# Attention softmax: exponential and row sums in one ScalarE instruction from PSUM, earlier q and k loads, fewer idle products

## What is computed

```python
scores = scale * np.matmul(q, k.transpose(0, 1, 3, 2))
mask_local = (rel >= 0) & (rel < 32)
mask_strided = (rel >= 0) & (pos[None, :] % 32 == pos[:, None] % 32)
# heads 0 to 3 local, 4 to 7 strided
scores = np.where(masks[None, :, :, :], scores, -1000000000.0)
scores = scores - scores.max(-1, keepdims=True)
attn = np.exp(scores)
attn = attn / (attn.sum(-1, keepdims=True) + 1e-09)
out = np.matmul(attn, v)
...
x = out as (2304, 512)
x = _moe_ref(x, w_in, w_out)        # dense MLP, 512 -> 2048 -> 512
return _moe2_ref(x, ...)            # top 2 of 8 experts
```

## Time and profile before

| | us |
|---|---|
| median of 3 runs | 1051.08 |
| lowest, highest | 1049.96, 1051.63 |
| the profiled execution | 1052.52 |
| its span, first to last instruction | 1050.9 |
| attention, up to the hand-over to the MLP | to about 194 of the span |

### The profile page before, as it was taken

The page is one execution under the profiler, slowest core; times in us unless marked ns, Lnnn a source line. Parts: engine busy times, 40 slices in busy tenths (PEclk is TensorE's granted clock), DMA queues, the critical chain, the costliest instruction groups (busy, mean ns, idle before and its releaser), DMA issues.

```text
span 1050.9 us, 22945 instructions
## 1 busy us (share of the span) xinstructions
PE 985.4 (94%) x9218; PEld 712.4 (68%) x9219; DVE 592.9 (56%) x1031; ACT 306.6 (29%) x426; POOL 223.2 (21%) x276
## 2 busy tenths in 40 slices
PE   7799999999999999999997779999999999999993
PEld 4677777767667577676763547767777776767671
DVE  5588997678678777787787362232323232323231
ACT  2345744523333243233441301111111111111110
POOL 4112313000000000020017032233332323232331
PEclk8699999999999999999998889999999999999997
DMA  9764581196857766667545823756565656565331
GB/s 259 177 173 98 129 204 38 46 377 208 258 174 220 262 234 205 226 214 261 179 142 177 280 49 99 183 164 193 153 188 151 181 158 185 161 189 157 81 76 34
DMA packets 170240, 182.43 MB, mean 174 GB/s; under 512 B 133495, under 2 KB 133495, under 8 KB 167360
## 3 DMA queue, kind: packets, MB, share of 16 engines
q1 hardware_dynamic: 112832, 142.47, 43.8%
q0 software_dynamic: 9600, 27.69, 8.8%
q10 hardware_dynamic: 47744, 11.35, 6.2%
HBM read 116.41 MB, written 53.55 MB: 162 GB/s over the span
## 4 chain that ended last, share of the span: by engine, by line
PE 78%; DVE 6%; DMA 4%; ACT 3%; SPq 2%; issue 2%; POOL 2%; ACTq 0%; POOLq 0%; DVEq 0%
PE bank L1748 18%; PE bank L1757 18%; PE bank L1576 16%; PE bank L1649 14%; PE bank L1552 4%; PE bank L1514 3%; PE bank L1484 2%; PE bank L1526 1%; DMA arena<-out,arena 1%; DMA out<-arena 1%; PE bank L1533 1%; DMA arena<-x_rows,arena 1%; DVE sc L965 1%; POOL x L645 1%; PE bank L1503 1%
## 5 line engine op out<-in xcount | busy, mean ns | idle before, releaser
L1576 PE MATMUL bank<-x,w_in_s 128*128 128x256 f16 (+1 forms) x1728 | 195.7, 274 | 3.2 <-ACT arena L790 2.1
L1649 PE MATMUL bank<-w_out_s,arena 128*128 128x512 f16 x864 | 190.3, 379 | 0.5 <-DVE arena L1121 0.5
L1576 PEld LDWEIGHTS bank<-x,w_in_s 128*128 128x128 f16 x1728 | 168.7, 98 | 27.4 <-issue 3.6
L1649 PEld LDWEIGHTS bank<-w_out_s,arena 128*128 128x128 f16 x864 | 83.6, 98 | 97.8 <-DVE arena L1121 1.0
L1420 DVE TENSOR_TENSOR arena<-arena 128x512 f32<-128x512 f32 x37 | 25.6, 692 | 165.6 <-ACT arena L896 105.0
L1748 PEld LDWEIGHTS bank<-arena,w_out_s 128*128 128x128 f16 x2016 | 114.5, 98 | 6.0 <-issue 1.0
L1748 PE MATMUL bank<-arena,w_out_s 128*128 128x128 f16 x2016 | 117.0, 219 | 0.6 <-issue 0.6
L1757 PE MATMUL bank<-w_in_s,arena 128*128 128x512 f16 x480 | 109.3, 385 | 7.2 <-DVE arena L1415 7.2
L1748 PEld LDWEIGHTS bank<-arena,w_in_s 128*128 128x128 f16 x1920 | 111.4, 99 | 5.6 <-DMA arena<-arena 0.5
L1748 PE MATMUL bank<-arena,w_in_s 128*128 128x128 f16 x1920 | 113.9, 221 | 0.7 <-DMA arena<-arena 0.4
L1757 PE MATMUL bank<-w_out_s,arena 128*128 128x512 f16 x480 | 106.9, 379 | 1.7 <-DVE arena L1415 1.7
(11 more groups left out here) (196 smaller groups left out, 1000.5 us busy)
## 6 DMA issues: line engine op xcount, KB each, us to landing
arena<-in_moe_w SPq DMA_DIRECT2D x16, 2048.0 KB, 11.8
split_weights<-arena SPq DMA_DIRECT2D x16, 2048.0 KB, 7.4
w_in_s<-split_weights SPq DMA_DIRECT2D x32, 512.0 KB, 4.2
w_out_s<-split_weights SPq DMA_DIRECT2D x32, 512.0 KB, 4.1
arena<-in_q SPq DMA_DIRECT2D x32, 144.0 KB, 3.2
arena<-in_k SPq DMA_DIRECT2D x32, 144.0 KB, 3.3
out<-zeros SPq DMA_DIRECT2D x1, 4608.0 KB, 24.7
x_rows<-arena SPq DMA_DIRECT2D x18, 256.0 KB, 3.2
```

The source lines that it names most:

```text
L1576: last = mm(dst, w_in_s[:, w_part, c, f * P:(f + 1) * P], x1[:, x_part, c, tok], start=(c == 0 and w_part + x_part == 0), stop=(c == DC - ...
L1649: last = mm(ps_x[j], g[par][:, g_part, f, j * P:(j + 1) * P], w_out_s[:, w_part, f], start=(n == 0), stop=(n == 3 * FC - 1))
```

## The change

The exponential reads the scores from PSUM. The maximum, times minus the scale, goes in as a bias for each row (`bias`, new, written by VectorE after the maximum). Since a bias holds for one block, there is one ACTIVATE for each block, and each writes the row sums of its block (`accum_out`). The subtraction, the buffer `lp` and the separate row sums are gone; VectorE's `sums` becomes `inverse`, which only inverts. What waited for `sub_done` now waits for `exp_done`: the scores that overwrite `ps_s`, and the first MLP product. Loads of q and k wait for the transposes of the pair that used the buffer before (`t_done`), and the v load behind them for a product (`pv_done`). At the start, the loads of pair 2 stand ahead of the second big load of v. The spread of v's maximum moves from the scores of half 0 to those of half 1. There are two idle products where there were four, and new ones of 512 columns between the first transposes and scores.

```diff
-            load_v(sp, 0, 0)
...
+            load_v(sp, 0, 0)
+            sp.wait_ge(S["t_done"], 4)
+            load_qk(0, 2)
             sp.dma_start(w_out_s[:]... v[2:4] ...).then_inc(S["v_flat_in1"], 16)
...
-                sp.wait_ge(S["s_done"], i * 2 + 2)
-                load_qk((i + 2) // PAIRS, (i + 2) % PAIRS)
+                if i > 0:
+                    sp.wait_ge(S["t_done"], 8 if i == 1 else 8 * i - 2)
+                    load_qk((i + 2) // PAIRS, (i + 2) % PAIRS)
+                wait(sp, S["pv_done"], i * 2 - 2)
                 load_v(sp, (i + 2) // PAIRS, (i + 2) % PAIRS)
...
-                act.wait_ge(S["sub_done"], (b * PAIRS + hp) * 2 + h2 + 1)
-                nc.scalar.activation(prob[hp % 2][h2][0:nq, 0:nb * nk], lp[h2][0:nq, 0:nb * nk], ACT.Exp,
-                                     scale=SCALE).then_inc(S["exp_done"], 1)
+                act.wait_ge(S["bias_done"], (b * PAIRS + hp) * 2 + h2 + 1)
+                half = nb // 2
+                for n in range(nb):
+                    at = n % half * nk
+                    last = nc.scalar.activation(prob[hp % 2][h2][0:nq, n * nk:(n + 1) * nk],
+                                                ps_s[h2][0:nq, n // half, at:at + nk], ACT.Exp,
+                                                bias=bias[0:nq, h2, n:n + 1], scale=SCALE,
+                                                accum_out=rs[0:nq, h2, n:n + 1])
+                last.then_inc(S["exp_done"], 1)
...
-                nc.vector.tensor_tensor(
-                    lp[h2][0:nq, 0:nb * nk].rearrange("p (a n k) -> p a n k", a=2, n=nb // 2), s_ps, m_b,
-                    ALU.subtract).then_inc(S["sub_done"], 1)
+                nc.vector.tensor_scalar(bias[0:nq, h2, 0:nb], mx[0:nq, h2, 0:nb], -SCALE, None, ALU.mult
+                                        ).then_inc(S["bias_done"], 1)
...
-                    pe.wait_ge(S["sub_done"], i * 2 + h2 - 1)
+                    pe.wait_ge(S["exp_done"], i * 2 + h2 - 1)
...
-                busy(4, slice(SEQ // 2, 4 * P))
+                busy(2, slice(SEQ // 2, 4 * P))
...
+            busy(2)
             pe.wait_ge(S["consts_pool"], 10)
             scores(0, 0, 0, 2)
+            busy(2)
             scores(0, 0, 1, 2)
+            busy(2)
...
+            busy(2)
             scores(0, 1, 0, 4)
+            busy(2)
             scores(0, 1, 1, 4)
+            busy(4)
...
-                    pe.wait_ge(S["sub_done"], 2 * NPAIR)
+                    pe.wait_ge(S["exp_done"], 2 * NPAIR)
```

More of the change, by code:

```diff
@@ L147, in program @@
         vn = [ca(F32, SB, 2, HD) for _ in range(PAIRS)]
-        lp = [ca(F32, LB * LK) for _ in range(2)]
         prob = [[ca(F32, LB * LK) for _ in range(2)] for _ in range(2)]
@@ L155, in program @@
         mx = ca(F32, 2, SB)
+        bias = ca(F32, 2, SB)
         rs = ca(F32, 2, SB)
@@ L282, in program @@
         ps_busy = bank[:, 6]
-        ps_all = ps_s[0][:, 0, 3 * P:4 * P]
+        ps_all = [t[:, 0, 3 * P:4 * P] for t in ps_s]
         ps_unit = bank[:, 6, 0:P]
@@ L980, in _, with max_and_bias @@
                       for t in (w_in_s, w_out_s)]
-            def max_and_sub(b, hp, h2, all_of=None):
+            def max_and_bias(b, hp, h2, all_of=None):
                 nq, nk, nb = geometry(hp)
@@ L988, in max_and_sub, with inverse @@
                 if all_of is not None:
-                    nc.vector.tensor_reduce(col(all_of), ps_all, AX.X, ALU.max).then_inc(S["all_max"], 1)
+                    nc.vector.tensor_reduce(col(all_of), ps_all[h2], AX.X, ALU.max).then_inc(S["all_max"], 1)
                 dve.wait_ge(S["mx_done"], n)
-                m_b = mx[0:nq, h2, 0:nb].rearrange("p (a n) -> p a n", a=2).unsqueeze(3).to_broadcast(
-                    [nq, 2, nb // 2, nk])
-                nc.vector.tensor_tensor(
-                    lp[h2][0:nq, 0:nb * nk].rearrange("p (a n k) -> p a n k", a=2, n=nb // 2), s_ps, m_b,
-                    ALU.subtract).then_inc(S["sub_done"], 1)
-            def sums(b, hp, h2):
-                nq, nk, nb = geometry(hp)
-                n = (b * PAIRS + hp) * 2 + h2 + 1
-                pr = prob[hp % 2][h2][0:nq, 0:nb * nk].rearrange("p (n k) -> p n k", n=nb)
-                dve.wait_ge(S["exp_done"], n)
-                nc.vector.tensor_reduce(rs[0:nq, h2, 0:nb], pr, AX.X, ALU.add).then_inc(S["sum_done"], 1)
-                dve.wait_ge(S["sum_done"], n)
+                nc.vector.tensor_scalar(bias[0:nq, h2, 0:nb], mx[0:nq, h2, 0:nb], -SCALE, None, ALU.mult
+                                        ).then_inc(S["bias_done"], 1)
+            def inverse(b, hp, h2):
+                nq, nk, nb = geometry(hp)
+                dve.wait_ge(S["exp_done"], (b * PAIRS + hp) * 2 + h2 + 1)
                 nc.vector.reciprocal(rr[hp % 2][0:nq, h2, 0:nb], rs[0:nq, h2, 0:nb]).then_inc(S["rr_done"], 1)
@@ L1018, in v_max @@
                 steps[0] += 1
-            max_and_sub(0, 0, 0)
-            max_and_sub(0, 0, 1)
+            max_and_bias(0, 0, 0)
+            max_and_bias(0, 0, 1)
             v_max(0)
-            sums(0, 0, 0)
-            sums(0, 0, 1)
+            inverse(0, 0, 0)
+            inverse(0, 0, 1)
             v_max(1)
-            max_and_sub(0, 1, 0)
-            max_and_sub(0, 1, 1)
+            max_and_bias(0, 1, 0)
+            max_and_bias(0, 1, 1)
             v_max(2)
@@ L1093, in stage_a @@
                     if more1:
-                        sums(b1, hp1, 0)
-                        sums(b1, hp1, 1)
+                        inverse(b1, hp1, 0)
+                        inverse(b1, hp1, 1)
                     if i == 0:
@@ L1101, in stage_a @@
                     if more2:
-                        max_and_sub(b2, hp2, 0, ALL_OF.get(i))
+                        max_and_bias(b2, hp2, 0, ALL_OF.get(i))
+                    if i > 0:
+                        out_lo(b, hp)
+                    if more2:
+                        max_and_bias(b2, hp2, 1, V_ALL if i == 0 else None)
                     if i == 0:
@@ L1105, in stage_a @@
                         power_of_two(col(V_ALL), col(S_V), col(I_V), step).then_inc(S["scaled"], 1)
-                    out_lo(b, hp)
-                    if more2:
-                        max_and_sub(b2, hp2, 1)
+                        out_lo(b, hp)
                     weights(b * PAIRS + hp)
@@ L1497, in scores @@
                     pe.wait_ge(S["raw_max"], maxima)
-                    mm(ps_all, top_of(column), identb[:], start=True, stop=True, skip_group_check=True)
+                    mm(ps_all[h2], top_of(column), identb[:], start=True, stop=True, skip_group_check=True)
                 mask = mask_l if is_local(hp) else mask_s
@@ L1615, in stage_a @@
                         scores(b2, hp2, 0, k[2] + 1,
-                               (V_MAX, 1) if hp == 0 else (B_MAX, b + 2) if hp == 1 else None)
+                               (B_MAX, b + 2) if hp == 1 else None)
                     else:
@@ L1620, in stage_a @@
                     if more:
-                        scores(b2, hp2, 1, k[2] + 1)
+                        scores(b2, hp2, 1, k[2] + 1, (V_MAX, 1) if hp == 0 else None)
                     else:
```

4 lines of the change are left out of this document (2 added, 2 removed).

## The result

The changed kernel takes 1110.43 us (median of 4 runs, 1102.89 to 1113.16) against 1050.52 us, a ratio of 1.057 with an interval of 1.050 to 1.063: 60 us slower. The profiled execution took 1108.37 us, its span is 1106.5 us, 55.6 more than before.

A forecast was written before the change was run, and what follows sets the result against it. TensorE bounds attention now, waiting only for ScalarE, which the change makes the bound. Span 1050.9 + 34 (pairs) + 5 (hand-over) - 3 (front) + 30 (clock) = 1116.9, so 1117 us; range 1060 to 1155, the forecast's own 1098 to 1145.

The forecast's parts named there:

- pairs 1 to 13 at the full clock: Attention pairs 1 to 13: longer exponentials make ScalarE the bound, 163.0 us for 128.7, 34 us more.
- low clock in them: Pairs 1 to 13: new gaps drop TensorE's clock in 7 of 13 pairs, 4.4 us each, 30 us more.
- loads past the front: Pairs past the front: asking for q and k at a transpose changes nothing, as no pair there waits for loads.
- front, to pair 1: Start of attention: the 7.8 us wait for pair 2's q and k goes, exponentials come late; 3 us less.
- hand-over: Attention to first MLP: its first product waits for the last two halves of exponentials, 5 us more (bounds 1.7 and 6.7).
- What bounds the kernel: Attention pairs: TensorE waits only for ScalarE's evacuations, nothing waits for VectorE, so relieving VectorE gains nothing.
- The price of a block: ScalarE's exponential with its read: 0.47 us (128 columns), 0.42 (72); bounds 0.26 and 0.21 with read hidden, 0.57 and 0.52.
- The loop: Each attention pair: ScalarE's evacuations and exponentials close a loop of 6.2 (local) or 5.8 us (strided) plus two exponential halves.
- a pair of 12 to 13 us where the clock is full: Sign in the profile after that the forecast is right: attention pairs this long at full clock, some 16 or 17 at low.
- The rival in which the clock holds: Attention: ScalarE is the bound but the clock stays full, 1087 us (1070 to 1098); chance 0.26.
- The faster rival: Attention: the read costs nothing, blocks under 0.28 (local) or 0.21 us (strided), 1045 us; chance 0.14.
- an ACTIVATE with its read under 0.3 us: Sign in ScalarE's profile after that the forecast is wrong and the read costs nothing, the change being faster.

The follow-up runs named there:

- a_oldloads: The changed kernel with SyncE's loads in the order and behind the waits of the kernel before: 1102.9 us.
- a_idle4: The changed kernel with four idle products ahead of each product with v instead of two: 1087.6 us.
- a_noacc: The changed kernel without row sums in the exponential's instruction; VectorE sums the probabilities again behind the exponentials: 1065.8 us.
- b_blocks: The kernel before with two idle products for four and its exponential cut into blocks with accumulator reads, from SBUF: 1077.9 us.
- b_early: The kernel before with two idle products for four, and q and k of pairs 2 and 3 loaded ahead of v of pair 2: 1062.6 us.
- b_idle2: The kernel before with two idle products ahead of each product with v instead of four: 1041.7 us, ratio 0.991 to 0.997.

## Why the prediction came out near

The forecast was 1117 us, the result is 1110.4. In the profiled spans, the terms are these. Pairs 1 to 13 run from 38.63 to 226.96, 188.3 us, for 128.7. At the full clock they would take 141 us: by kind 10.6, 10.97, 10.44 and 10.07 us for hp 1, 2, 3 and 0 (pair 5 here, pairs 10 to 12 of a_oldloads), and 1.0 for each of the four weight splits (pair 9 of a_idle4 takes 11.64 for 10.6). What is left, less the wait for a load, is put down to the low clock.

| term | predicted | measured |
|---|---|---|
| pairs 1 to 13 at the full clock | +34 | +12.3 (141 - 128.7) |
| low clock in them | +30 | +43.5 (the rest) |
| loads past the front | 0 | +3.8 |
| front, to pair 1 | -3 | -6.5 |
| hand-over | +5 | +4.3 (6.1 - 1.8) |
| sum | +66 | +57.4 |

The spans differ by 55.6, so behind the hand-over 1.8 us less are left. Two terms were wrong by 22 and 14 us, with opposite signs, so that the sum came within 7 us is in part luck.

**What bounds the kernel: right.** Relieving VectorE paid nothing; giving it the sums back in a_noacc made the kernel faster, and pair 5 takes 10.60 us with two idle products, with four and with nine more.

**The price of a block: mis-sized.** The failed step is that the read "may overlap a neighbour by the 0.10 that those two do". It overlaps by much more: start to start 0.343 and 0.295 us for my 0.47 and 0.42, nearer the lower bound of 0.26 and 0.21. By that bound's own definition, the read hidden, a_noacc shows 0.21 us for 72 columns, so the bound was exact there, and the read adds 0.08.

The Trainium skill (ScalarE: Activation LUTs, Rules for kernel authors) by its budget gave 0.41 and 0.36 us without the read. The measured 0.343 and 0.295, with the read, are below it.

**The loop: right in form.** Two halves plus 6.2 or 5.8 us, with the measured blocks, is 77.8 + 24.7 + 33.0 + 4.4 = 139.9 us, 10.8 a pair, as measured. (24.7 is 72 blocks of 0.343 us, 33.0 is 112 of 0.295.) With the block's price the sign "a pair of 12 to 13 us where the clock is full" failed too: it is 10.1 to 11.0, and 11.6 with a weight split. The two waits stood where they were expected, at 0.89 and 0.43 us in place of 1.5 each.

**The clock: right in kind and count, wrong in price.** The pair at the low clock takes 16.83 us, predicted 16.9. But a low pair costs the distance from the loop to this figure, and with the loop at 10.8 that is 6.0 us, for the 4.4 that I had. 43.5 / 6.0 is 7 pairs, and by the mean clock of 0.63 it is 8; I took 7, as a choice between none and thirteen and no derivation, so the count is luck. The two errors share their source: what a shorter loop saves at the full clock, the low clock takes back, because TensorE's own work sets the low pair. Pair 3, 7 or both take the same 16.83 us in a_noacc, a_oldloads, b_blocks and b_early, whose pairs differ at the full clock, and 17.57 in a_idle4 with its two idle products more. The spans times their mean clocks are close too, 1010 us for the changed kernel (1106.5 x 0.913), 1011 for a_noacc (1063.5 x 0.951), 1006 for b_idle2 (1040.5 x 0.967). That fits, but proves nothing. Why the clock falls at one dip and not at the next like it stays open.

By the rule of the Trainium skill (TensorE: Matmul & The Clock Gate, Why this matters for your kernels) this term was zero; the rows at 118 to 122, with no wait in the two pairs ahead of them above 0.9 us, are against it. The rival in which the clock holds gave 1087, 23 below the result.

**Front and loads.** "The first P transpose comes at 25.7 and q of pair 2 at 26.8" was right (26.21, 27.33). "From there to 45.11 I leave the distance" was not: this stretch took 11.3 us for 15.1, part of it now at the full clock. Wrong too was the 0 for loads past the front, taken from "no row of a pair past the front waits for a load". That holds for the rows before; but SP's queue needs 7.22 us to issue v of pair 2, pair 3's q and k are behind it, and a front that is 6.5 us shorter wants them 6.5 us sooner. I had not counted that piece of the queue.

**The hand-over** held: an exponential releases it, 4.3 us for the 6 that I had before taking off 1.0 for idle products. The 16 blocks took 4.9 us (228.03 to 232.93) for 6.7. What follows took 1.8 us less, for the 1.0.

**The faster rival** needed blocks under 0.28 and 0.21 us; they are not. I had also written that an ACTIVATE with its read under 0.3 us would speak for it. Strided blocks are under that, at 0.295, and the rival is still wrong, so that sign was set too high.

## What to carry to other kernels

Cutting one long ScalarE instruction into many and adding a read to each costs little by itself. It matters through what is queued behind it on ScalarE: count the evacuations that TensorE waits for, before the load on the relieved engine. In this loop 0.9 us a pair was worth 11 us by itself and 45 in all, so ask of each edit what it does to TensorE's gaps, take several executions, and look at the mean clock of each one before believing a small gain. Moving a load earlier only helps until the next load behind it in the issuing queue is wanted; where that was mended too (b_early), the gain of 3.4 us was lost again in five of six executions, when the clock fell.

## What was not expected of the hardware

- The accumulator read has a row of 225 to 236 ns (mean) but adds 0.08 us to the start-to-start time: 0.295 for about 0.21 us at 72 columns from PSUM with a bias. From SBUF without a bias the pair of instructions takes 0.245 us.
- The clock falls behind dips that most pairs pass without a fall (0.76 and 0.80 busy in two rows), and executions of one kernel then lie up to 42 us apart (b_early, 1037.9 at 0.970, 1080.0 at 0.925). Even the kernel before has single executions at 1067 to 1080 us with clocks of 0.934 to 0.948.
- Fewer idle products can be faster or slower than more in the same loop: of 4, 2 and 0 ahead of each product the kernel before takes 1050, 1042 and 1061 us; with the new exponential 4 beat 2 by 23 us.
